# Where the last pass of a fused attention and mixture-of-experts kernel reads its eight tile numbers, transposes its first rows and signals the end of an expert

## The chip, the cores and the metric

The kernel runs on one core of a Trainium2 chip. The metric is the device time of one execution in microseconds, the median of several executions. One execution was also taken with the hardware profiler, and all rows below come from it.

A core has a matrix engine (PE; its weight loads are listed as PEld), a vector engine (DVE), a scalar engine (ACT), a general engine (POOL) and a queue engine (SP) that only starts transfers here. Each engine has a sequencer of its own, which reads its instructions in order; PEldq, DVEq, ACTq and SPq in a row stand for work of the sequencer alone: register arithmetic, branches, waits and loads of a number into a register.

## The reference

Three layers, in float32. N = 2304 tokens, width 512.

```python
scores = scale * np.matmul(q, k.transpose(0, 1, 3, 2))      # attention with a block mask
attn = np.exp(scores - max); attn = attn / (sum + 1e-9)
x = np.matmul(attn, v)                                      # to (2304, 512)
h = x @ w_in                                                # 512 -> 2048
x = np.maximum(0.01 * h, h) @ w_out                         # 2048 -> 512
do_compute = x @ w_skip > 0                                 # tokens that go to an expert
e_idx = np.argmax(x @ w_gate, axis=1)                       # one of 8 experts
h = np.maximum(xc[mask] @ w1[e], 0.0)                       # 512 -> 1024, expert e
y[mask] = gate_w[mask, None] * (h @ w2[e])                  # 1024 -> 512
out[do_compute] = xc + y                                    # the others keep x
```

## The kernel before, in words

Each engine has its own instruction list, and the lists meet only through semaphores: `wait_ge(s, n)` holds an engine until the counter `s` has reached `n`, and `then_inc` or `sem_inc` raises it. The order of the work is the order in which it is written.

Attention, the two projections and the gate take the first 640 us. After them the tokens of each expert lie in tiles of 128 rows. How many tiles an expert has is known only at run time. DVE therefore works out nine tile numbers (`base_i`, raised with `s_count`), and each engine reads all nine into registers: `tile_start(e, x)` is one such load, `tile_starts(e)` waits for `s_count` and does all nine. `starts[x]` to `starts[x + 1]` are then the bounds of a loop over the tiles of expert x, which each engine runs on its own. With this input the eight loops have 11 turns in all; the first expert has three, and one more tile, the early one, goes ahead of them.

- The **early tile** (`early_hidden`, `early_y`): PE multiplies its 128 tokens with both weights of expert 0. `early_y(f)`, f = 0 to 7, is one product of 512 columns, in `ps_y`; the last one raises `m_y` to 1.
- **A tile of the loops**, number g. POOL gathers its token rows from memory into `rows` (`m_gather`). PE transposes them (`transpose_rows(g)`, `m_rt`), DVE copies the transposed rows out of PSUM (`move_rows_t(g)`, L1286, `m_rows`), PE makes the hidden layer in two halves (L1612, `ps_hid`, `m_hid`), ACT rounds each half (`hid_hi`, `m_high`), DVE takes what rounding left (`hid_lo`, L1306, `m_low`), PE makes the second product out of hi and lo parts (L1623 to L1625, `ps_y`, `m_y`), DVE forms the result (`y_out`, `m_out`), POOL scatters it. The transposes of tile g + 1 stand between the two products of tile g.
- **Once for each expert** ACT rounds its second weight in four pieces (`high_w2`, L986), and DVE takes the rest in four pieces (`low_w2`, L1291). The rounded weight has one buffer for all experts, so ACT waits until the last product of the expert before is done, for which it reads `m_y`. At the same place it raises `s_expert`, on which SP waits before it loads the weights of expert x over those of x - 4. SP has two weight transfers under way at a time.

Of the kernel before, what the change touches and what calls it, by code (L numbers as in the profile page):

```python
# [15 lines left out]
P = 128  # L16
# [3 lines left out]
KC = DM // P  # L20
# [3 lines left out]
EC = F // P  # L24
# [121 lines left out]
def build(nc, q_t, k_t, v_r, w_in, w_out, w_gs, w1, w2, out):  # L146
    ctx = ExitStack()
    with ctx:
        def sb(name, shape, dt=F32, scope=ctx):
            return scope.enter_context(nc.sbuf_tensor(name, shape, dt))  # L150

        def ps(name, cols, scope=ctx):
            return scope.enter_context(nc.psum_tensor(name, [P, cols], F32))

        def sem(name):
            return ctx.enter_context(nc.semaphore(name))
# [6 lines left out]
        ident = sb("ident", [P, P])  # L163
# [104 lines left out]
        rows = sb("rows", [P, ROW_W])  # L268
# [30 lines left out]
        ps_rt = ps("ps_rt", BANK)  # L299
# [65 lines left out]
        s_ready = sem("s_ready")  # L365
        s_count = sem("s_count")
        s_order = sem("s_order")
        s_w = [[sem(f"s_w{i}{n}") for n in range(2)] for i in range(NW)]
        s_expert = sem("s_expert")
# [4 lines left out]
        m_gather = sem("m_gather")  # L374
        m_sidx = sem("m_sidx")
        m_scatter = sem("m_scatter")
        m_rt = sem("m_rt")
# [6 lines left out]
        m_y = sem("m_y")  # L384
# [85 lines left out]
        def loaded_to(e, x, n):  # L470

            for k, loaded in enumerate(s_w[x % NW]):
                e.wait_ge(loaded, 16 * (W_LOADS // 2 * (x // NW) + (n + 2 - k) // 2))
# [16 lines left out]
        def tile_start(e, x):  # L490
            return e.value_load(base_i[0:1, x:x + 1], min_val=0, max_val=MAX_TILES)

        def tile_starts(e):
            e.wait_ge(s_count, 1)
            return [tile_start(e, x) for x in range(E + 1)]
# [354 lines left out]
        def _(e):  # L850
# [77 lines left out]
            for s in range(STEPS):  # L928
# [14 lines left out]
                f, odd = divmod(s - 42, 2)  # L943
# [33 lines left out]
                e.copy(held[:, :], rows[:, :]).then_inc(m_held, 1)  # L977

            def high_w2(x, n):
                if n == 0 and x >= 1:  # L980

                    e.wait_ge(m_y, starts[x] + 1)
                    e.sem_inc(s_expert, 1)
                e.wait_ge(s_w2lo, W2_PIECES * x)
                loaded_to(e, x, KC + n)
                e.activation(w2_hi[:, 2 * n:2 * n + 2, :], w2_sb[x % NW][:, 2 * n:2 * n + 2, :], ACT.Copy).then_inc(s_w2hi, 1)  # L986
# [12 lines left out]
            starts = tile_starts(e)  # L999
# [17 lines left out]
        def _(e):  # L1017
# [266 lines left out]
            def move_rows_t(g):  # L1284
                e.wait_ge(m_rt, g + 1)
                e.tensor_copy(rows_t[:, :, :].rearrange("p k c -> p (k c)"), ps_rt[:, :]).then_inc(m_rows, 1)  # L1286

            def low_w2(x, n):
# [2 lines left out]
                e.tensor_tensor(w2_lo[x % NW][:, fs, :], w2_sb[x % NW][:, fs, :], w2_hi[:, fs, :].bitcast(F32),  # L1291
                                ALU.subtract).then_inc(s_w2lo, 1)

            starts = tile_starts(e)
            move_rows_t(0)
            e.wait_ge(m_y, 1)
            e.scalar_tensor_tensor(out=y_out[:, :], in0=ps_y[:, :], scalar=early[:, DM:DM + 1],
                                   in1=early[:, 0:DM], op0=ALU.mult, op1=ALU.add).then_inc(m_out, 1)
            for x in range(E):
                for n in range(W2_PIECES):  # L1300
                    low_w2(x, n)
                with e.Fori(starts[x], starts[x + 1]) as g:
                    for half in range(2):
                        fs = slice(EC // 2 * half, EC // 2 * (half + 1))
                        e.wait_ge(m_high, 2 * g + half + 2)
                        e.scalar_tensor_tensor(out=hid_lo[:, fs, :].rearrange("p f c -> p (f c)"), in0=ps_hid[half][:, :],  # L1306
                                               scalar=0.0, in1=hid_hi[:, fs, :].rearrange("p f c -> p (f c)").bitcast(F32),
                                               op0=ALU.max, op1=ALU.subtract).then_inc(m_low, 1)
                    move_rows_t(g + 1)
                    e.wait_ge(m_y, g + 2)  # L1310
                    e.wait_ge(m_kept, g + 2)
                    e.wait_ge(m_scatter, (g + 1) * 16)
                    e.scalar_tensor_tensor(out=y_out[:, :], in0=ps_y[:, :], scalar=kept[:, DM:DM + 1],
                                           in1=kept[:, 0:DM], op0=ALU.mult, op1=ALU.add).then_inc(m_out, 1)
# [3 lines left out]
        def _(e):  # L1318
# [221 lines left out]
                    if n % (EC // 2 * KC) == EC // 2 * KC - 1:  # L1540
                        last.then_inc(s_earlyhid, 1)

            def transpose_rows(g):
                e.wait_ge(m_gather, (g + 1) * 16)
                for c in range(KC):
                    last = e.transpose(ps_rt[:, P * c:P * c + P], rows[:, P * c:P * c + P], ident[:, :])
                last.then_inc(m_rt, 1)

            def early_y(f):

                if f == 0:
# [37 lines left out]
            tabulate(m)  # L1589
            early_hidden(27, EC * KC)  # L1590

            starts = []
            for f in range(EC):
                if f == EC - 1:
                    e.wait_ge(s_ready, 1)
                    transpose_rows(0)
                early_y(f)
                if f == 0:
                    e.wait_ge(s_count, 1)
                starts.append(tile_start(e, f))  # L1600
            starts.append(tile_start(e, E))

            for x in range(E):
                i = x % NW
                with e.Fori(starts[x], starts[x + 1]) as g:
                    e.wait_ge(m_rows, g + 1)
                    loaded_to(e, x, KC - 1)
                    e.wait_ge(m_low, 2 * g + 1)
                    for half in range(2):
                        for f in range(EC // 2 * half, EC // 2 * (half + 1)):  # L1610
                            for c in range(KC):
                                last = e.matmul(ps_hid[half][:, P * f - HALF * half:P * (f + 1) - HALF * half],  # L1612
                                                w1_sb[i][:, c, P * f:P * f + P], rows_t[:, c, :],
                                                start=c == 0, stop=c == KC - 1)
                        last.then_inc(m_hid, 1)
                    transpose_rows(g + 1)
                    e.wait_ge(m_out, g + 1)
                    for f in range(EC):
                        if f % 2 == 0:
                            e.wait_ge(s_w2lo, W2_PIECES * x + f // 2 + 1)  # L1620
                        if f % (EC // 2) == 0:
                            e.wait_ge(m_low, 2 * g + f // (EC // 2) + 2)
                        e.matmul(ps_y[:, :], hid_hi[:, f, :], w2_hi[:, f, :], start=f == 0, stop=False)  # L1623
                        e.matmul(ps_y[:, :], hid_hi[:, f, :], w2_lo[i][:, f, :], start=False, stop=False)  # L1624
                        last = e.matmul(ps_y[:, :], hid_lo[:, f, :], w2_hi[:, f, :], start=False, stop=f == EC - 1)  # L1625
                    last.then_inc(m_y, 1)


_NAMES = ("q_t", "k_t", "v_r", "w_in", "w_out", "w_gs", "w1", "w2")
# [24 lines left out]
```

## Time and profile before

| | |
|---|---|
| median of three executions | 800.74 us (799.68 to 808.11) |
| the profiled execution, its own time | 800.74 us |
| its span, first to last instruction | 798.5 us |
| PE busy | 762.1 us (95%) |
| DVE, ACT, POOL busy | 381.4, 308.4, 165.2 us |
| granted TensorE clock, mean | 0.997 of full speed |

The span is what the trace shows; the 2.2 us around it belong to the time as well. The profiled execution has the median's time. A busy share says only how much of the span an engine had work; what an edit is worth depends on which wait ends last at its place.

### The profile page before, as it was taken

To read this page: it belongs to the slowest core of one execution; us is meant where nothing else is said; L and a number is where in the kernel's file an instruction comes from. 1 tells how busy PE (TensorE), PEld (TensorE's weight loads), DVE (VectorE), ACT (ScalarE), POOL (GpSimd) and SP (SyncE) were. 2 spreads that over 40 slices of the span, in tenths; PEclk is the share of its full clock that TensorE was granted. 3 is DMA by queue.
4 is the path that set the end of the run, shared out by engine and by line. 5 is a ranking of instruction groups with operands and counts; after the bars stand their busy time and mean duration, and the time that the engine had idled before them with its cause. 6 is when DMAs were issued, how large, how long until landed. Compare 5 with 4: busy or idle time off the path is not lost.

```text
span 798.5 us, 13602 instructions
## 1 busy us (share of the span) xinstructions
PE 762.1 (95%) x4690; PEld 654.8 (82%) x4690; DVE 381.4 (48%) x790; ACT 308.4 (39%) x723; POOL 165.2 (21%) x201
## 2 busy tenths in 40 slices
PE   4887899999999999999999999999999999999997
PEld 3665688888988888899998778787787879999996
DVE  4878555543342464112344555655554341444554
ACT  3656656544443445334342222222321131333533
POOL 5344656321211223200020000000000032222222
PEclk9999999999999999999999999999999999999999
DMA  5646677754544443265766565565652137777750
GB/s 147 169 136 189 180 192 205 205 150 113 140 131 129 126 141 87 75 190 156 191 191 180 159 186 152 169 198 151 180 155 84 54 91 239 241 227 232 232 176 4
DMA packets 101623, 126.84 MB, mean 159 GB/s; under 512 B 15938, under 2 KB 62290, under 8 KB 101560
## 3 DMA queue, kind: packets, MB, share of 16 engines
q1 hardware_dynamic: 98392, 121.37, 52.3%
q0 software_dynamic: 2080, 3.77, 1.5%
q10 hardware_dynamic: 1088, 0.89, 0.5%
q8 instruction: 36, 0.59, 0.3%
q14 instruction: 27, 0.22, 0.1%
HBM read 92.89 MB, written 31.57 MB: 156 GB/s over the span
## 4 chain that ended last, share of the span: by engine, by line
PE 88%; DMA 4%; SPq 4%; issue 1%; ACT 1%; DVE 1%; POOL 0%; POOLq 0%; DVEq 0%; ACTq 0%
PE ps_hid L1612 10%; PE ps_h L1404 9%; PE ps_x L1454 9%; PE ps_x L1456 8%; PE ps_x L1455 8%; PE ps_h L1406 8%; PE ps_h L1405 8%; PE ps_o L1388 5%; PE ps_t L1362 3%; PE ps_y L1624 3%; PE ps_y L1625 3%; PE ps_y L1623 3%; PE ps_s L1347 2%; DMA k<-k_st 2%; PE ps_s L1348 2%
## 5 line engine op out<-in xcount | busy, mean ns | idle before, releaser
L1404 PE MATMUL ps_h<-xh,win_h 128*128 128x384 f32 x384 | 136.4, 355 | 3.0 <-ACT act L891 2.4
L1405 PE MATMUL ps_h<-xl,win_h 128*128 128x384 f32 x384 | 128.8, 336 | 0.0
L1406 PE MATMUL ps_h<-xh,win_l 128*128 128x384 f32 x384 | 128.8, 335 | 0.0
L1454 PE MATMUL ps_x<-wout_h,g_hi 128*128 128x512 f32 x288 | 117.0, 406 | 0.0
L1456 PE MATMUL ps_x<-wout_h,g_lo 128*128 128x512 f32 x288 | 112.5, 391 | 0.0
L1455 PE MATMUL ps_x<-wout_l,g_hi 128*128 128x512 f32 x288 | 112.2, 390 | 0.0
L891 ACT ACTIVATE act<-ps_h 128x384 f32<-128x384 f32 x96 | 47.1, 491 | 151.1 <-PE ps_h L1406 151.1
L1044 DVE COPY pt<-ps_t 128x256 f32<-128x256 f32 (+4 forms) x113 | 49.2, 443 | 107.0 <-PE ps_t L1362 106.8
L1078 DVE TENSOR_TENSOR g_lo<-g_raw,g_hi 128x512 fp32r<-128x512 f32 x72 | 49.6, 688 | 76.0 <-ACT g_hi L901 75.9
L879 ACT ACTIVATE prob<-ps_s,neg_max 128x128 f32<-128x128 f32 (+2 forms) x144 | 78.3, 547 | 9.3 <-DVE neg_max L1038 9.3
L1612 PEld LDWEIGHTS ps_hid<-rows_t,w_sb 128*128 128x128 f32 x704 | 80.2, 192 | 1.7 <-issue 0.8
L1404 PEld LDWEIGHTS ps_h<-xh,win_h 128*128 128x128 f32 x384 | 72.1, 188 | 10.8 <-issue 5.4
L1612 PE MATMUL ps_hid<-rows_t,w_sb 128*128 128x128 f32 x704 | 80.5, 275 | 0.0
L1038 DVE TENSOR_REDUCE neg_max<-ps_s 128x1 f32<-128x128 f32 (+2 forms) x144 | 71.7, 502 | 8.7 <-PE ps_s L1348 8.7
L705 POOL TENSOR_TENSOR k_st<-k_raw,k_st 64x576 fp32r<-64x576 f32 x32 | 45.6, 1426 | 142.6 <-DVE k_st L1024 142.3
L1405 PEld LDWEIGHTS ps_h<-xl,win_h 128*128 128x128 f32 x384 | 72.3, 188 | 0.0
L1406 PEld LDWEIGHTS ps_h<-xh,win_l 128*128 128x128 f32 x384 | 72.1, 188 | 0.0
L1456 PEld LDWEIGHTS ps_x<-wout_h,g_lo 128*128 128x128 f32 x288 | 54.1, 188 | 11.9
L1454 PEld LDWEIGHTS ps_x<-wout_h,g_hi 128*128 128x128 f32 x288 | 54.2, 188 | 11.7 <-issue 2.2
L1455 PEld LDWEIGHTS ps_x<-wout_l,g_hi 128*128 128x128 f32 x288 | 54.2, 188 | 9.5
L1347 PE MATMUL ps_s<-k_st,q_hi 128*128 128x128 f32 (+3 forms) x128 | 46.6, 364 | 15.5 <-POOL ident L733 10.8
L1362 PE MATMUL ps_t<-ident,prob 128*128 128x128 f32 x344 | 60.5, 279 | 0.7 <-ACT prob L879 0.7
(176 smaller groups left out, 1134.9 us busy)
## 6 DMA issues: line engine op xcount, KB each, us to landing
w_sb<-in_w SPq DMA_DIRECT2D x64, 512.0 KB, 5.4
hidden<-act SPq DMA_DIRECT2D x96, 192.0 KB, 2.5
g_raw<-hidden SPq DMA_DIRECT2D x72, 256.0 KB, 4.3
k_raw<-in_k_t SPq DMA_DIRECT2D x62, 144.0 KB, 3.0
q_raw<-in_q_t SPq DMA_DIRECT2D x32, 144.0 KB, 3.2
x2rows<-x SPq DMA_DIRECT2D x18, 256.0 KB, 2.5
out<-x SPq DMA_DIRECT2D x18, 256.0 KB, 2.7
k<-k_st SPq DMA_DIRECT2D x31, 144.0 KB, 2.8
```

The costliest lines, as they stand in the source:

```text
L879: e.activation(prob_of(u), score_out(u), ACT.Exp, bias=neg_max[:, u % 4:u % 4 + 1], scale=1.0, accum_out=row_sum[p % 2][:, i:i + 1]).then_ ...
L1038: e.tensor_reduce(out=neg_max[:, u % 4:u % 4 + 1], in_=src, axis=AX.XY if u % UNITS == TAIL else AX.X, op=ALU.max, negate=True).then_inc(s ...
L1078: e.tensor_tensor(g_lo[j % G_RING][:, :, :], g_raw[j % RAW_RING][:, :, :], g_hi[j % G_RING][:, :, :].bitcast(F32), ALU.subtract).then_inc( ...
L1347: e.matmul(dst, q_hi[h][:, P * qt:P * qt + P], k_st[h][:, 0:cols], start=True, stop=False)
L1362: last = e.transpose(t_bank(u, P, P * kt, P * kt + P), tile[:, P * kt:P * kt + P], ident[:, :])
L1404: e.matmul(dst, win_h[:, f, kc, :], xh[slot][:, kc, :], start=kc == 0, stop=False)
L1405: e.matmul(dst, win_h[:, f, kc, :], xl[slot][:, kc, :], start=False, stop=False)
L1406: last = e.matmul(dst, win_l[:, f, kc, :], xh[slot][:, kc, :], start=False, stop=kc == KC - 1)
L1454: e.matmul(dst, hi, wout_h[:, f, :], start=f == 0, stop=False)
L1455: e.matmul(dst, hi, wout_l[:, f, :], start=False, stop=False)
L1456: last = e.matmul(dst, lo, wout_h[:, f, :], start=False, stop=f == FC - 1)
L1612: last = e.matmul(ps_hid[half][:, P * f - HALF * half:P * (f + 1) - HALF * half], w1_sb[i][:, c, P * f:P * f + P], rows_t[:, c, :], start= ...
```

## The change

Three things.

1. PE now does the wait for `s_count` ahead of the first `early_y`, reads all its tile numbers behind the eight `early_y`, one behind each, and does the first `transpose_rows(0)` after all of these. Before, that transposition stood ahead of the last `early_y`.
2. DVE reads its nine tile numbers behind `move_rows_t(0)` and the first `y_out`. Before, it read them first of all.
3. The end of an expert is signalled by PE: behind the loop of each expert it waits until its own last product is done (`m_y`) and raises `s_expert`. ACT, which did both, now waits on `s_expert` ahead of each piece of `high_w2`.

```diff
@@ ACT
             def high_w2(x, n):
-                if n == 0 and x >= 1:
-                    e.wait_ge(m_y, starts[x] + 1)
-                    e.sem_inc(s_expert, 1)
+                e.wait_ge(s_expert, x)
                 e.wait_ge(s_w2lo, W2_PIECES * x)
@@ DVE
-            starts = tile_starts(e)
             move_rows_t(0)
             e.wait_ge(m_y, 1)
             e.scalar_tensor_tensor(out=y_out[:, :], in0=ps_y[:, :], scalar=early[:, DM:DM + 1],
                                    in1=early[:, 0:DM], op0=ALU.mult, op1=ALU.add).then_inc(m_out, 1)
+            starts = tile_starts(e)
             for x in range(E):
@@ PE
+            e.wait_ge(s_count, 1)
             starts = []
             for f in range(EC):
-                if f == EC - 1:
-                    e.wait_ge(s_ready, 1)
-                    transpose_rows(0)
                 early_y(f)
-                if f == 0:
-                    e.wait_ge(s_count, 1)
                 starts.append(tile_start(e, f))
             starts.append(tile_start(e, E))
+            e.wait_ge(s_ready, 1)
+            transpose_rows(0)
             for x in range(E):
...
                     last.then_inc(m_y, 1)
+                e.wait_ge(m_y, starts[x + 1] + 1)
+                e.sem_inc(s_expert, 1)
```

DVE's instructions from the last tile number worked out to the second weight of expert 0, before. TENSOR_LOAD with two ISA rows is one `tile_start`, and nine of them stand in a row.

```order
L1282 CAST base_i<-base_f 128x9 [waits s_t]
L491 TENSOR_LOAD base_i [waits s_count]
L491 ISA x2
...
L1286 COPY rows_t<-ps_rt 128x512 [waits m_rt]
L1297 SCALAR_TENSOR_TENSOR y_out<-ps_y,act 128x512 [waits m_y]
L1291 TENSOR_TENSOR w_lo<-w_sb,w_hi 128x1024 [waits s_w2hi] x4
```

The same place of the changed kernel:

```order
L1279 CAST base_i<-base_f 128x9 [waits s_t]
L1283 COPY rows_t<-ps_rt 128x512 [waits m_rt]
L1293 SCALAR_TENSOR_TENSOR y_out<-ps_y,act 128x512 [waits m_y]
L491 TENSOR_LOAD base_i [waits s_count]
L491 ISA x2
...
L1288 TENSOR_TENSOR w_lo<-w_sb,w_hi 128x1024 [waits s_w2hi] x4
```

The nine loads have moved from ahead of the copy and `y_out` to between `y_out` and the second weight's first piece.

PE's instructions from the last product of expert 0 to the first of expert 1, before. REGISTER_ALU and COMPARE_AND_BRANCH end the loop, the branch and the two ISA rows begin the next one.

```order
L1625 MATMUL ps_y<-w_hi,hid_lo 128x512
L1605 REGISTER_ALU
L1605 COMPARE_AND_BRANCH
L1605 UNCONDITIONAL_BRANCH
L1605 ISA
L1608 ISA [waits s_w11,s_w10,m_rows]
L1612 MATMUL ps_hid<-rows_t,w_sb 128x128 [waits m_low]
```

The same place of the changed kernel:

```order
L1620 MATMUL ps_y<-w_hi,hid_lo 128x512
L1600 REGISTER_ALU
L1600 COMPARE_AND_BRANCH
L1622 REGISTER_ALU
L1600 UNCONDITIONAL_BRANCH [waits m_y]
L1600 ISA
L1603 ISA [waits s_w11,s_w10,m_rows]
L1607 MATMUL ps_hid<-rows_t,w_sb 128x128 [waits m_low]
```

A wait on `m_y`, which the MATMUL four rows above it raises, now stands between the two products, at each of the eight ends of an expert.

## Rows read from the trace of the kernel before

**Rows 1.** The page, part 4: the chain that ended last, by engine.

```profile
PE 88%; DMA 4%; SPq 4%; issue 1%; ACT 1%; DVE 1%; POOL 0%; POOLq 0%; DVEq 0%; ACTq 0%
```

**Rows 2.** The view by stretches: from the second tile's first product to the last's.

```profile
core 0: us, PE busy (x) PEld busy (x) DVE busy (x) ACT busy (x) POOL busy (x), PEclk, DMA share, GB/s
661.78:780.04 118.26, 118.26 (x831) 108.83 (x830) 51.81 (x60) 43.08 (x60) 25.70 (x36) 1.00 0.70 224
```

**Rows 3.** The timeline from 640 to 656 us: start, length, engine, instruction.

```profile
640.30 0.60 ACT L990 ACTIVATE hid_early<-ps_hid 128x512 f32<-128x512 f32 x1 [3.51 <-PE ps_hid L1537]
...
647.55 0.69 DVE L1286 COPY rows_t<-ps_rt 128x512 f32<-128x512 f32 x1 [6.88 <-PE ps_rt L1546]
...
648.38 7.22 PEld L1612 LDWEIGHTS ps_hid<-rows_t,w_sb 128*128 128x128 f32 x64 [0.83 <-issue]
...
648.41 0.75 DVE L1297 SCALAR_TENSOR_TENSOR y_out<-ps_y,act 128x512 f32<-128x512 f32 x1 [0.17 <-PE ps_y L1556]
...
649.08 4.62 DVE L1291 TENSOR_TENSOR w_lo<-w_sb,w_hi 128x1024 fp32r<-128x1024 f32 x4
...
653.62 0.69 DVE L1306 SCALAR_TENSOR_TENSOR hid_lo<-ps_hid,hid_hi 128x512 fp32r<-128x512 f32 x1
...
655.96 0.19 PEld L1623 LDWEIGHTS ps_y<-w_hi,hid_hi 128*128 128x128 f32 x1
```

**Rows 4.** The chain from 640 us in order of time: start, length, what.

```profile
647.51 0.86 PE ps_y L1556 x2
648.38 7.41 PE ps_hid L1612 x64
...
780.04 7.14 PE ps_hid L1612 x64
```

**Rows 5.** Line L491, the register loads: ns min/median/max, first and last start us.

```profile
L491 ACTq TENSOR_LOAD <-base_i x9: 272/275/472, 640.7 to 645.2; - x9
...
L491 DVEq TENSOR_LOAD <-base_i x9: 297/304/547, 640.7 to 645.9; - x9
...
L491 DVEq SEQ_ASSERT  x9: 23/23/35, 641.5 to 646.5; - x9
```

**Rows 6.** The timeline of ACT and of DVE in the last tile.

```profile
780.24 3.90 ACT L986 ACTIVATE w_hi<-w_sb 128x1024 fp32r<-128x1024 f32 x4 [5.06 <-PE ps_y L1625]
...
783.61 2.35 DVE L1291 TENSOR_TENSOR w_lo<-w_sb,w_hi 128x1024 fp32r<-128x1024 f32 x2
...
787.85 0.69 DVE L1306 SCALAR_TENSOR_TENSOR hid_lo<-ps_hid,hid_hi 128x512 fp32r<-128x512 f32 x1 [1.29 <-ACT hid_hi L1010]
```

**Rows 7.** Sequencer work by line, columns as in Rows 5; x1: of a short stretch.

```profile
L1285 DVEq ALU_OP  x11: 40/40/40, 656.5 to 787.9; - x11
L1302 DVEq MOVE  x1: 36/36/36, 784.2 to 784.2; - x1
L983 ACTq EVENT_SEMAPHORE  x7: 17/17/17, 688.1 to 780.1; - x7
L1544 PEldq EVENT_SEMAPHORE  x1: 51/51/51, 645.7 to 645.7; - x1
L1605 PEldq MOVE  x8: 29/37/37, 647.2 to 776.0; - x8
L1608 PEldq FUSED_REGOPS  x11: 37/37/47, 648.3 to 776.3; - x11
```

**Rows 8.** The timeline of PE at 82 us, in the attention.

```profile
82.85 0.76 PE L1337 MATMUL ps_s<-k_st,q_hi 128*128 128x288 f32 x4 [3.73 <-DMA k<-k_st]
```

**Rows 9.** PE's waits over the whole span: total us, times, longest us.

```profile
PE ps_s L1337 <- DMA k<-k_st: 9.7, 4, 3.7
```

**Rows 10.** The view by stretches, the 4 us after that wait, columns as in Rows 2.

```profile
84.00:88.00 4.00, 4.00 (x19) 1.97 (x16) 1.85 (x5) 3.49 (x10) 3.14 (x3) 0.57 0.50 153
```

**Rows 11.** Line L592, all weight loads of the experts.

```profile
L592 SPq DMA_DIRECT2D w_sb<-in_w x64: 327/328/1269, 413.4 to 772.0; - x64
...
DMA to landing us min/median/max: 4.2/5.4/10.0
```

More of the change, by code:

```diff
@@ L1541, in early_hidden @@
                         last.then_inc(s_earlyhid, 1)
[L1543 to L1547, printed above, removed]
             def early_y(f):
@@ L1590, in _, with transpose_rows @@
             early_hidden(27, EC * KC)
+            e.wait_ge(s_count, 1)
             starts = []
             for f in range(EC):
-                if f == EC - 1:
-                    e.wait_ge(s_ready, 1)
-                    transpose_rows(0)
                 early_y(f)
-                if f == 0:
-                    e.wait_ge(s_count, 1)
                 starts.append(tile_start(e, f))
             starts.append(tile_start(e, E))
+            def transpose_rows(g):
+                e.wait_ge(m_gather, (g + 1) * 16)
+                for c in range(KC):
+                    last = e.transpose(ps_rt[:, P * c:P * c + P], rows[:, P * c:P * c + P], ident[:, :])
+                last.then_inc(m_rt, 1)
+            e.wait_ge(s_ready, 1)
+            transpose_rows(0)
             for x in range(E):
```

## The prediction, made before the changed kernel ran

> **What bounds the kernel now.** The chain that ended last is PE for 88% [rows 1], so I read next whether PE has any room where the change touches it. The view by stretches says no: from the second tile's first product to the last tile's PE is busy 118.26 us of 118.26 [rows 2], at the full clock. The reader is to see that here any time in which PE does nothing is added to the end, however short it is, unless a later wait would have eaten it. The expert pass has no such wait in PE's rows. Then I read the timeline around the first tile, for who releases whom [rows 3], the chain for what a product costs in the middle and after a pause [rows 4], and the sequencers' own rows, which busy time doesn't count [rows 5, 7], because two of the three edits move sequencer work and the third adds a sequencer wait.
>
> **1. PE's early tile.** Before, PE transposes the rows, then does the last `early_y`, and under that product (0.86 us in the chain, [rows 4]) DVE copies the rows out. The copy begins at 647.55 and takes 0.69; PE's first weight load of the hidden layer follows at 648.38, 0.83 behind the copy's start [rows 3]. That is nearly as long as the cover, so the copy costs little today. Afterwards all eight `early_y` come first, so the transposes end 0.86 later, and nothing stands on PE over the copy: its start moves to 647.55 + 0.86 = 648.41, PE's load to 648.41 + 0.83 = 649.24. The earlier wait on `s_count` adds a trifle. It is satisfied at about 640.7, when all sequencers begin to load [rows 5], and before it held the first register load, now the first `early_y` with that load right behind it; I put 0.05 us on it. The other loads run on PE's sequencer under the products, as they do now. Sum for this edit: 0.86 + 0.05 = **0.9 us**, all on the path.
>
> **2. DVE's nine loads.** They last from 640.7 to 646.5 [rows 5], 5.8 us. Before, they lie in DVE's wait of 6.88 us for the transposes [rows 3], so they cost nothing. What covers them is that wait, and the change takes them out of it. Behind them on DVE stand the four pieces of `w_lo` (649.08 to 653.62, where `hid_lo` follows at once) and then `hid_lo` of the first half, 0.69 us, for which PE's second product waits; PE came to it at 655.96 and did not have to wait [rows 3]: 655.96 - (653.62 + 0.69) = 1.65 us of room.
>
> When do the loads begin now? Two questions, two rows. Does DVE's sequencer pass an instruction whose wait isn't satisfied yet? The register step L1285 stands behind the second `hid_lo` of a tile, which waits for ACT; it ran at 787.9 in the last tile, where that `hid_lo` began at 787.85 after an idle 1.29 us [rows 6, 7]. It did not run during the idle time. So no: the loads can't begin before the copy is released. Does it run ahead of instructions that are released, but have not begun? The MOVE of L1302 behind the four pieces ran at 784.2 [rows 7], when ACT's fourth piece had just ended (780.24 + 3.90 = 784.14) and DVE was still in the third of its own (783.61 + 2.35 for two, [rows 6]). So yes. ACT's first load, too, ran at 640.7 while its activation of 640.30 to 640.90 was under way [rows 3, 5]. Hence the loads begin right behind the copy's release, at about 648.41 + 0.05 + 0.05 = 648.5, and end at 648.5 + 5.8 = 654.3. ACT's pieces are long done by then, so the four pieces take the same 653.62 - 649.08 = 4.54, `hid_lo` runs from 658.85 to 659.55, and PE starts its second product some 0.05 later, at 659.6, instead of 655.96. **The first tile ends 3.65 us later**; this holds the 0.9 us of the first edit, since PE would have been there at 655.96 + 0.9 = 656.9 and stands for 2.7 us. Bounds: if the loads had to wait until DVE has finished the copy and `y_out`, they begin 0.69 + 0.75 = 1.4 later, and the tile 5.1 us later. If they ran before the release they cost nothing, and only 0.9 is left. I take 3.65, which both rows speak for. What follows in the tile has room: the other half is due 12 products later.
>
> The Trainium skill speaks against this sum. Its page "Perfetto Trace Analysis", section "DVE / Act Engine Instruction (TENSOR_ADD, Activation, etc)", has the sequencer push an instruction into a wait queue and read on before its semaphores are satisfied. By that rule the loads would still run in DVE's long wait and the first tile would lose only the 0.9 us. The row on L1285 disagrees, and I go by the row.
>
> **3. The end of an expert.** Before, PE's sequencer is through the loop's end 4 us ahead of its array: the MOVE that opens the last loop ran at 776.0, the product behind it has its slot at 780.04 [rows 4, 7]. So all this branching is hidden under products. Now the sequencer has to stand until its own last product has reached PSUM. ACT saw the same event at 780.1 at the last such place, and the next product's slot began at 780.04 [rows 4, 7]. From there in order: PE's wait (51 ns each on this engine, with its spacing about 0.1), from MOVE to the last register step 776.3 - 776.0 = 0.3, from there to the weight load 648.38 - 648.3 = 0.1 [rows 3, 7]. Weight load at 780.6, 0.56 late. And the array starts empty, with a weight load that nothing covers: the first hidden layer, which came after such a pause, took 7.41 where a running one takes 7.14, 0.27 more [rows 4]. Together 0.83, of times given to a tenth, so I say **0.8 us**. ACT's semaphore row has seven such places in it [rows 7]; the eighth, behind the last expert, has no product behind it. 7 x 0.8 = **5.6 us**. Lower bound: PE loses at least the 0.27 and the 0.06 to the event and the 0.1 of its wait, 0.43 each, 3.0. Upper bound: reading new code behind the wait, which no row shows at this place; I allow the register part once more, 0.3 each, 7.7.
>
> Who else waits? ACT gets its signal about 0.1 us later than now, since PE passes it on, and its four extra waits lie under activations of one microsecond. DVE's chain has room: in the last tile the pieces end at 785.96 and `hid_lo` at some 786.6, while PE's hidden layer ends at 780.04 + 7.14 = 787.2, with transposes still to do [rows 4, 6], and PE comes later now. SP's weight loads wait on `s_expert` too. Even if the whole delay went into them, the last would land at 772.0 + 9.3 + 10.0 = 791.3 [rows 11]; its user is the fourth piece of ACT, at 780.24 + 3 x 0.95 + 9.3 = 792.4. So it costs nothing. Taking ACT's wait away gives nothing back, since ACT wasn't late.
>
> **Sum.** 3.65 + 5.6 = 9.25, say 9.3 us. The profiled execution took 800.74, which is also the median: 800.7 + 9.3 = **810.0 us**, span 807.8. About 1% is what a measurement of this kernel can tell from no change; its threshold is 808.7.
>
> **Rivals.**
> A. The sequencer passes unreleased waits, by whatever it does where no row looks: 0.9 + 5.6 = 6.5, 807.2. Against it L1285.
> B. The end of an expert is cheaper than I add up, at its lower bound: 3.65 + 3.0 = 6.7, 807.4. For it: a branch that overlaps the end of the product. Against it: the steps are in order on one sequencer.
> C. The stall of 2.7 us, or of 4.1 if the loads begin late, makes the TensorE clock drop. Once PE stood idle for 3.73 us, and in the 4 us from 84 on the granted clock was 0.57 in the mean, for most of them the lower of its levels, 1.2 instead of 2.4 GHz; that is 0.43 x 4 = 1.7 us of full clock. The three other waits of that kind were 6.0 us together [rows 8 to 10], and the mean clock of 0.997 over the span leaves no room for a drop behind each. So with the drop 810.0 + 1.7 = 811.7; with the late loads 811.7 + 1.4 = 813.1.
> D. Not slower: the stream of expert weights, not PE, sets the end of the pass, so that every pause of PE is paid back in a wait that gets shorter. It would give 800.7. It decides from the point where a weight lands later than PE needs it; the last was issued at 772.0 and lands in 10.0 at worst, before ACT's fourth piece at 783.1 [rows 6, 11], and PE has no idle time at all in [rows 2]. Nearly excluded.
>
> **Chances.** Forecast 0.62 (own range 808.3 to 811.3), A 0.10, B 0.08, C 0.17, D 0.03. The range reaches down to just under A and B and up over C with early loads: 806.6 to 812.4, leaving out D and the late end of C. Slower by over 1%: nearly all of the forecast and C, 0.76; within 1%: A, B, D and the low end of the forecast, 0.23; faster by over 1%: 0.01.
>
> **What would show it.** In the trace after: DVE's L491 loads from about 648.5 to 654.3, none before the copy; PE's L1607 load at 649.3 and L1618 load near 659.6, behind `hid_lo`; the tiles of one expert still 13.1 us apart, and 13.9 where an expert ends between them, seven times; ACT's and DVE's work unchanged in length. I am wrong if PE's second product of the first tile starts before 658, if the steps between experts are under 13.6 or over 14.2, or if a PE wait turns up on a weight load.

## The result and the profile after

| | before | after |
|---|---|---|
| median of 17 executions each | 804.37 us (799.68 to 810.79) | 815.15 us (808.83 to 820.58) |
| ratio after to before, 95% interval | | 1.0131 [1.0095, 1.0168] |
| the profiled execution, its own time | 800.74 us | 815.26 us |
| its span | 798.5 us | 813.0 us |
| PE busy | 762.1 us | 769.2 us |
| granted TensorE clock over the span, mean | 0.997 | 0.988 |

The change makes the kernel slower by 1.3%. The forecast was +9.3 us, a ratio of 1.012. The ratio of 1.0131 on the median of 804.37 is +10.5 us, and the two medians lie 10.8 apart. The absolute forecast of 810.0 us and its range up to 812.4 were missed, because they stood on 800.7 for the kernel before, and its median over 17 executions is 804.4.

The profile of the changed kernel. The page, busy time and chain by engine, to be read beside [rows 1]:

```profile
PE 769.2 (95%) x4690; PEld 657.4 (81%) x4690; DVE 380.3 (47%) x790; ACT 309.1 (38%) x723; POOL 165.3 (20%) x201
...
PE 85%; SPq 4%; DMA 4%; issue 2%; DVE 2%; ACT 1%; POOL 1%; DVEq 1%; POOLq 0%; ACTq 0%
```

PE's share of the chain fell from 88% to 85%, and DVE, its sequencer and "issue" have a percent more each: the path to the end now leaves PE in places where it did not before.

The timeline around the first tile, to be read beside [rows 3]. Everything here starts some 5 us later than in the profile before; that arises ahead of everything that the change touches (below), so I read distances from the first row, in which DVE writes the tile numbers.

```profile
645.16 0.17 DVE L1279 CAST base_i<-base_f 128x9 int32<-128x9 f32 x1
...
653.09 0.69 DVE L1283 COPY rows_t<-ps_rt 128x512 f32<-128x512 f32 x1 [7.75 <-PE ps_rt L1593]
653.70 0.74 DVE L1293 SCALAR_TENSOR_TENSOR y_out<-ps_y,act 128x512 f32<-128x512 f32 x1
653.92 7.22 PEld L1607 LDWEIGHTS ps_hid<-rows_t,w_sb 128*128 128x128 f32 x64 [1.10 <-issue]
...
659.22 4.63 DVE L1288 TENSOR_TENSOR w_lo<-w_sb,w_hi 128x1024 fp32r<-128x1024 f32 x4 [4.78 <-issue]
663.77 1.28 DVE L1303 SCALAR_TENSOR_TENSOR hid_lo<-ps_hid,hid_hi 128x512 fp32r<-128x512 f32 x2
...
664.51 0.19 PEld L1618 LDWEIGHTS ps_y<-w_hi,hid_hi 128*128 128x128 f32 x1 [2.98 <-DVE hid_lo L1303]
664.51 0.50 PE L1618 MATMUL ps_y<-w_hi,hid_hi 128*128 128x512 f32 x1 [2.74 <-DVE hid_lo L1303]
```

Line L491, DVE's register loads, to be read beside [rows 5]:

```profile
L491 DVEq TENSOR_LOAD <-base_i x9: 298/311/555, 653.1 to 658.6; - x9
...
L491 DVEq SEQ_ASSERT  x9: 23/23/35, 653.9 to 659.1; - x9
```

The reader is to see the "4.78 <-issue" on `w_lo`: DVE's array stands still, waits for nothing that another engine owes it, and all the while its own sequencer loads numbers (653.1 to 659.1). Then `hid_lo` comes late and PE stands 2.74 us for it.

The chain at the ends of experts, start, length and what, to be read beside [rows 4], and PE's row for the new wait:

```profile
670.34 7.14 PE ps_hid L1607 x64
...
683.47 7.14 PE ps_hid L1607 x64
...
696.62 0.57 issue
697.19 7.41 PE ps_hid L1607 x64
...
710.59 0.57 issue
711.16 7.41 PE ps_hid L1607 x64
```

```profile
L1623 PEldq EVENT_SEMAPHORE  x8: 51/51/51, 696.6 to 807.8; - x8
```

The tiles of the first expert follow each other at once (670.34, 683.47: 13.13 apart, hidden layer 7.14). At an end of an expert stand 0.57 of "issue" and a hidden layer of 7.41. The view of waits for the same stretch sums it up (us in total, times, longest):

```profile
PE ps_hid L1607 <- PE ps_y L1620: 4.1, 7, 0.6
...
PE ps_y L1618 <- DVE hid_lo L1303: 2.7, 1, 2.7
```

**Where the time went.** To compare kernels whose expert pass begins at different times, I take one distance in every trace: from the start of `base_i` to the start of the last `y_out`. I call it the pass. Before it was 793.34 - 640.50 = 152.84 us:

```profile
640.50 0.17 DVE L1282 CAST base_i<-base_f 128x9 int32<-128x9 f32 x1
...
793.34 0.75 DVE L1313 SCALAR_TENSOR_TENSOR y_out<-ps_y,kept 128x512 f32<-128x512 f32 x1 [4.20 <-PE ps_y L1625]
```

After it is 807.85 - 645.16 = 162.69. The change therefore costs **9.85 us** in the rows, and the spans differ by 14.5 only because the profiled execution after reached `base_i` 4.66 later, in work that the change does not touch.

### The profile page after: what moved, and what is told of

Read it like the earlier page. It is cut to its first block, busy times and chain, and to the rows that moved or that the text cites. A ratio compares the mean times of both kernels' runs of the same rounds, so it can differ in the third digit from the quotient of the medians.

```text
span 813.0 us, 13636 instructions
## 1 busy us (share of the span) xinstructions
PE 769.2 (95%) x4690; PEld 657.4 (81%) x4690; DVE 380.3 (47%) x790; ACT 309.1 (38%) x723; POOL 165.3 (20%) x201
## 4 chain that ended last, share of the span: by engine, by line
PE 85%; SPq 4%; DMA 4%; issue 2%; DVE 2%; ACT 1%; POOL 1%; DVEq 1%; POOLq 0%; ACTq 0%
PE ps_hid L1607 9%; PE ps_x L1451 9%; PE ps_h L1401 9%; PE ps_x L1453 8%; PE ps_x L1452 8%; PE ps_h L1402 8%; PE ps_h L1403 8%; PE ps_o L1385 6%; PE ps_t L1359 3%; PE ps_y L1618 3%; PE ps_y L1620 3%; PE ps_y L1619 3%; PE ps_s L1344 2%; DMA k<-k_st 2%; PE ps_s L1345 2%
## 5 line engine op out<-in xcount | busy, mean ns | idle before, releaser
L1401 PEld LDWEIGHTS ps_h<-xh,win_h 128*128 128x128 f32 x384 | 72.1, 188 | 10.5 <-issue 4.7
```

The costliest lines, as they stand in the source:

```text
L1401: e.matmul(dst, win_h[:, f, kc, :], xh[slot][:, kc, :], start=kc == 0, stop=False)
```

## The experiments

All kernels start from the kernel before unless another is named. "Hidden" and "second" are PE's first hidden-layer load and its first second-product load of tile 0, counted from the start of `base_i`; "pass" is the distance above; "clock 0:100" is the granted clock in the first 100 us of the span.

| kernel | `base_i` | clock 0:100 | hidden | second | pass | over before | ratio of times [95%] |
|---|---|---|---|---|---|---|---|
| before | 640.50 | 0.98 | 7.88 | 15.46 | 152.84 | | |
| before_again | 644.49 | 0.91 | 7.79 | 15.37 | 152.76 | -0.08 | 0.9982 [0.9947, 1.0017] |
| after | 645.16 | 0.91 | 8.76 | 19.35 | 162.69 | 9.85 | 1.0131 [1.0095, 1.0168] |
| after_again | 646.48 | 0.90 | 8.67 | 19.26 | 162.63 | 9.79 | 1.0110 [1.0068, 1.0152] |
| pe_order | 650.22 | 0.86 | 8.66 | 16.24 | 153.63 | 0.79 | 1.0016 [0.9980, 1.0051] |
| dve_loads | 644.15 | 0.93 | 7.79 | 19.25 | 158.00 | 5.16 | 1.0084 [1.0046, 1.0122] |
| expert_end | 649.42 | 0.86 | 7.79 | 15.37 | 158.79 | 5.95 | 1.0081 [1.0050, 1.0112] |
| pe_dve | 640.27 | 0.98 | 8.66 | 19.26 | 158.24 | 5.40 | 1.0077 [1.0040, 1.0114] |
| pe_dve_again | 643.57 | 0.93 | 8.66 | 19.25 | 156.68 | 3.84 | one execution |
| met_wait | 646.01 | 0.91 | 7.79 | 15.37 | 152.80 | -0.04 | 1.0011 [0.9974, 1.0048] |
| every_tile | 640.32 | 0.97 | 7.79 | 15.36 | 164.11 | 11.27 | 1.0160 [1.0095, 1.0224] |
| fill_pauses | 648.64 | 0.95 | 7.78 | 15.36 | 152.80 | -0.04 | 1.0055 [1.0022, 1.0088] |
| early_cover | 643.94 | 0.95 | 6.94 | 15.09 | 152.47 | -0.37 | 0.9994 [0.9964, 1.0023] |

In the first profile of the kernel before, "hidden" is 7.88; in the six others that leave PE's early tile as it was it is 7.78 or 7.79. So a difference from that first profile is good to 0.1 us.

### pe_order: the first edit alone

```diff
+            e.wait_ge(s_count, 1)
             for f in range(EC):
-                if f == EC - 1:
-                    e.wait_ge(s_ready, 1)
-                    transpose_rows(0)
                 early_y(f)
-                if f == 0:
-                    e.wait_ge(s_count, 1)
                 starts.append(tile_start(e, f))
             starts.append(tile_start(e, E))
+            e.wait_ge(s_ready, 1)
+            transpose_rows(0)
```

> The kernel before with edit 1 alone: PE waits for s_count first, does all eight early_y and then the first transposes; DVE and the expert ends as before. I measure the expert stretch, from the start of DVE's last tile-number step (CAST base_i) to the start of the last y_out; it was 152.84 us before (640.50 to 793.34) and is 162.69 after the change (645.16 to 807.85). My theory (three local causes that add up): the stretch grows by 0.9 us, all of it ahead of the first hidden-layer product, so 153.7. Rival (the excess over the forecast comes from the code being laid out differently, anywhere): the stretch stays within 0.1 of a kernel without the edit and the time ahead of it moves. The whole time: within 1% of before.

Measured: the hidden layer begins 0.78 later from `base_i` (8.66 for 7.88), and the pass is 0.79 longer; 153.7 was expected, 153.63 measured. The timeline of this kernel:

```profile
658.06 0.69 DVE L1286 COPY rows_t<-ps_rt 128x512 f32<-128x512 f32 x1 [7.66 <-PE ps_rt L1546]
...
658.88 7.22 PEld L1610 LDWEIGHTS ps_hid<-rows_t,w_sb 128*128 128x128 f32 x64 [1.10 <-issue]
```

The load starts 0.82 behind the copy's start, nearly as before (0.83), but the product that used to run over the copy now lies ahead of it. By time alone the edit can't be told from nothing (1.0016).

### dve_loads: the second edit alone

```diff
-            starts = tile_starts(e)
             move_rows_t(0)
             e.wait_ge(m_y, 1)
             e.scalar_tensor_tensor(out=y_out[:, :], in0=ps_y[:, :], ...).then_inc(m_out, 1)
+            starts = tile_starts(e)
```

> The kernel before with edit 2 alone: DVE reads its nine tile numbers behind the first y_out. The transposes are released at 647.55 as before, so the loads run for 6.0 us (653.1 to 659.1 in the changed kernel) from there, w_lo starts at 653.6 instead of 649.08, the first hid_lo ends near 658.8 and PE, which came at 655.96, stands for 2.9 us. My theory: the stretch is 152.84 + 2.9 = 155.7. Rival (a sequencer reads past a wait that isn't met): loads while DVE waits, stretch 152.84. Second rival (the stall makes the TensorE clock drop): a lower granted clock in the 10 us behind the stall and a stretch of about 157.4.

Timeline and line L491 of this kernel:

```profile
644.15 0.17 DVE L1282 CAST base_i<-base_f 128x9 int32<-128x9 f32 x1
...
651.11 0.69 DVE L1286 COPY rows_t<-ps_rt 128x512 f32<-128x512 f32 x1 [6.78 <-PE ps_rt L1546]
...
651.97 0.75 DVE L1296 SCALAR_TENSOR_TENSOR y_out<-ps_y,act 128x512 f32<-128x512 f32 x1 [0.17 <-PE ps_y L1556]
...
658.11 4.63 DVE L1291 TENSOR_TENSOR w_lo<-w_sb,w_hi 128x1024 fp32r<-128x1024 f32 x4 [5.39 <-issue]
...
663.40 0.80 PE L1623 MATMUL ps_y<-w_hi,hid_hi 128*128 128x512 f32 x1 [3.61 <-DVE hid_lo L1306]
```

```profile
L491 DVEq TENSOR_LOAD <-base_i x9: 296/310/576, 652.0 to 657.5; - x9
```

The pass of 158.00 missed the expected 155.7 by 2.3 us. The second product comes 3.79 late, a microsecond more than this edit's share of the forecast, which is 3.65 less the 0.9 of the first edit; the other 1.37 is a drop of the clock (below, at pe_dve). The loads did not begin behind the copy (651.11) but at 652.0, when `y_out` was released. In PE's old order the last `early_y`, for which `y_out` waits, ends 0.86 behind the copy's release; in the new order it ends ahead of it. So the loads begin 7.9 us behind `base_i` with or without the first edit, and the second product comes 19.25 or 19.26 behind it. **The two edits do not add**: 0.78 and 3.79 alone, 3.80 together.

These rows also decide whether the sequencer passes an instruction whose wait is unmet. DVE waited 6.78 us for the transposes with the loads third in its list, the tile numbers were ready (PE's own loads of them began at 644.4), and not one load ran until both waits ahead were satisfied; then the first of them began, under the execution of `y_out`.

### expert_end: the third edit alone

```diff
@@ ACT
-                if n == 0 and x >= 1:
-                    e.wait_ge(m_y, starts[x] + 1)
-                    e.sem_inc(s_expert, 1)
+                e.wait_ge(s_expert, x)
@@ PE
                     last.then_inc(m_y, 1)
+                e.wait_ge(m_y, starts[x + 1] + 1)
+                e.sem_inc(s_expert, 1)
```

> The kernel before with edit 3 alone: PE waits for its own last product at the end of each expert and raises s_expert; ACT waits on s_expert. My theory: each of seven ends costs 0.84 us (0.57 of pause and 0.27 of a product that starts from an empty array, as in the changed kernel), stretch 152.84 + 5.9 = 158.7. Rival (in the changed kernel part of the cost came from ACT or DVE being late after the first tile's stall): under 0.6 each, stretch below 157. If edits 1 and 2 give 0.9 and 2.9, then the three sum to 9.7 against 9.85 measured.

The chain of this kernel, at the last of seven such ends ("issue" is 0.56 to 0.60 at all seven):

```profile
794.06 0.59 issue
794.65 7.41 PE ps_hid L1609 x64
```

The pass is 5.95 longer and the first tile unchanged; 5.95 / 7 = 0.85 for each end. Sum of the parts: 3.80 + 5.95 = 9.75, and the whole change measured 9.85 and 9.79. No part of the change gives anything back.

### before_again: the same kernel once more

> The kernel before, unchanged, timed and profiled once more. In the changed kernel's profile the stretch accounts for 9.85 us of the 14.5 us between the spans; the other 4.66 lie ahead of it, in code that the change doesn't touch, with 17 us at half clock in the first 100 us where the profile of before has 3.4. My theory (that part is chance, from run to run): the unchanged kernel shows it too: its stretch is 152.8 again, while its start of the stretch differs from 640.5 by some microseconds and follows the granted clock of the first 100 us. Rival (the change caused it): the stretch starts at 640.5 within 0.5 again.

The view by stretches, 0 to 100 us, of the kernel before and of this run (columns as in [rows 2]), and the timeline's row of `base_i` in this run:

```profile
0.00:100.00 100.00, 74.49 (x479) 57.18 (x481) 67.12 (x155) 57.46 (x162) 47.65 (x58) 0.98 0.59 164
```

```profile
0.00:100.00 100.00, 76.08 (x448) 57.14 (x449) 64.74 (x149) 53.45 (x151) 44.95 (x55) 0.91 0.55 152
```

```profile
644.49 0.17 DVE L1282 CAST base_i<-base_f 128x9 int32<-128x9 f32 x1
```

The program is the same; one execution got through 479 matmuls in the first 100 us at a clock of 0.98, the other through 448 at 0.91, and reached `base_i` 3.99 later. The pass itself is the same to 0.08. So two profiled executions of one kernel differ by 4 us ahead of the change's place, and the profile on which I forecast was the earlier of the two.

The traces also show where the difference arises. In none of the thirteen profiles is the clock under 1.00 between 100 us and `base_i`, and in the first 100 us it is so only in stretches that begin within 2 us of the end of one of the four pauses that PE makes between 38 and 92 us, waits for `k` as in [rows 8] (three of the four in fill_pauses have another cause). In the first profile of the kernel before, the pauses of 2.16, 1.98 and 1.83 us had no such stretch behind them and the one of 3.73 us had [rows 10]. In pe_order, whose program is the same up to there, the pauses were 2.11, 2.44, 2.27 and 2.90 us, and the view by stretches behind the four is:

```profile
40.40:44.40 4.00, 4.00 (x17) 3.35 (x19) 1.49 (x4) 2.10 (x6) 1.18 (x2) 0.50 0.31 97
57.40:61.40 4.00, 4.00 (x17) 3.33 (x19) 1.51 (x4) 2.17 (x7) 1.25 (x2) 0.50 0.30 87
74.20:78.20 4.00, 3.97 (x17) 3.36 (x19) 1.46 (x4) 2.16 (x7) 0.87 (x3) 0.50 0.51 146
92.00:96.00 4.00, 4.00 (x17) 3.30 (x19) 1.54 (x4) 3.25 (x9) 2.83 (x4) 0.50 0.39 108
```

All four run at the lower level, 1.2 GHz, and that execution reached `base_i` 9.72 us later than the first.

### pe_dve and pe_dve_again: the first two edits together, twice

> The kernel before with edits 1 and 2 together, expert ends as before. Alone, edit 1 made the stretch 153.62 (0.8 more) and edit 2 made it 158.00 (5.2 more, of which PE's second product starts 3.8 later, and the rest is a half-clock interval behind a pause of 3.6 us). My theory now: edit 2 alone has its loads held not by the copy but by y_out, whose release is the last early_y, 0.86 after the transposes; edit 1 puts y_out's release ahead of the copy's, so that the two together cost less than edit 2 alone: PE's second product 19.3 us after CAST base_i, a pause of 2.7 us, stretch 152.84 + 3.9 = 156.8, no half clock behind it. Rival (the costs add up): 0.8 + 3.8 = 4.6, stretch 157.4 or more, pause 3.6.

> The kernel with edits 1 and 2, one more profile. By the theory that the pause of 2.7 us drops the clock only in some executions: stretch 158.2 with a half-clock interval in the expert pass, or 156.8 (steps of y_out 17.0 instead of 18.4 at the first tile) without one. Either way PE's second product 19.26 us after CAST base_i.

Both have the second product at 19.25 or 19.26, as expected, and PE's pause of 2.75 and 2.74. But the pass was 5.40 longer in one (158.24 for the expected 156.8) and 3.84 in the other. The view by stretches behind the pause, first of pe_dve, then of pe_dve_again:

```profile
661.00:665.00 4.00, 4.00 (x12) 3.12 (x11) 0.00 (x0) 0.00 (x0) 0.06 (x1) 0.57 0.85 261
```

```profile
664.00:668.00 4.00, 4.00 (x19) 3.23 (x18) 0.00 (x0) 0.00 (x0) 0.35 (x2) 1.00 0.79 254
```

In the first the clock was 0.57 in the mean, 1.2 GHz for most of those 4 us (12 matmuls for 19); in the second it stayed at 1.00. That is 5.40 - 3.84 = 1.56 us. In dve_loads, where PE stood 3.61, it fell too (0.58 in the mean from 663.4 to 667.0): 5.16 - 3.79 = 1.37 of that kernel's pass. In the two profiles of the whole change it stayed at 1.00. A drop behind the pause of 2.7 us was seen in one of four profiles.

### met_wait and every_tile: what the end of an expert costs by itself

Both add to the kernel before a wait and a signal that nobody needs, the first of an event that is long past, the second behind every tile of its own last product.

```diff
@@ PE, met_wait: behind the loop of each expert
+                e.wait_ge(m_y, starts[x + 1])
+                e.sem_inc(s_idle, 1)
@@ PE, every_tile: last in the body of the loop
                     last.then_inc(m_y, 1)
+                    e.wait_ge(m_y, g + 2)
+                    e.sem_inc(s_idle, 1)
```

> The kernel before, to which PE does at each expert's end the same steps as in edit 3, a register step, a wait on m_y and a sem_inc (on a semaphore that nobody reads), but waits for one tile less, starts[x + 1] instead of starts[x + 1] + 1, which has been done for 13 us. ACT signals s_expert as before. It tells the drain from the steps. My theory (PE has to stand until its own last product has come out, and the loop's steps then stand bare): nothing, steps of 13.14 between all tiles, stretch 152.8. Rival (the added instructions, or code fetched anew, cost on their own): 0.2 to 0.84 at each of seven ends, stretch 154 to 158.7.

> The kernel before, to which PE waits for its own last product at the end of every tile instead of every expert (m_y at g + 2, then a sem_inc nobody reads). ACT signals s_expert as before, so that ACT isn't in the relay. Ten ends have a product behind them instead of seven. My theory: 0.84 us each, 8.4 in all, stretch 161.2, also in the first expert, whose three tiles are 13.13 apart today and then 13.97. Rival (it is the start of a new loop, not the drain, that costs): nothing at the turns inside a loop; ends of experts 0.84, stretch 158.7. Since the turn of a loop has fewer steps than the start of one, a turn may be up to 0.2 cheaper.

The chain of met_wait, whose third row is the first tile behind the end of an expert, then of every_tile:

```profile
667.25 7.14 PE ps_hid L1613 x64
...
680.39 7.14 PE ps_hid L1613 x64
...
693.52 7.14 PE ps_hid L1613 x64
```

```profile
648.11 7.41 PE ps_hid L1613 x64
...
661.52 0.98 issue
662.50 7.41 PE ps_hid L1613 x64
...
675.91 0.85 issue
676.76 7.41 PE ps_hid L1613 x64
```

With a wait that is already met the tiles stay 13.13 apart and the pass is unchanged, though there are as many added instructions as in expert_end. With the wait on its own product inside the loop, ten places cost 11.27, 1.13 each, for the expected 0.84. So what costs is the standstill: PE's array runs empty, and the wait, the registers and the branch come one after the other behind the last product. All ten places are dearer than the 0.56 to 0.60 of "issue" in expert_end: 0.98, 0.85 and 0.86 at the three turns inside a loop, 0.79 to 0.96 at the seven ends of experts. Here the loop's own counting and branching stand behind the wait (661.7 and 661.9 in PE's sequencer, the wait at 661.5), while in expert_end they stand ahead of it. That this order makes the difference is read from the rows; no kernel changed it alone.

### fill_pauses: something for PE to do in the attention's pauses

```diff
@@ PE, scores(u): ahead of the waits for the next head's k
+                if i == TAIL and 1 <= p <= 4:
+                    e.wait_ge(s_exp, s_freed(u))
+                    c = BANK * (s_slot(u) % S_RING)
+                    for _ in range(8):
+                        e.matmul(ps_s[:, c:c + P], ident[:, :], ident[:, :], start=True, stop=True)
```

The added products compute nothing that is used.

> The kernel before, with eight unneeded 128-column products of ident on PE ahead of the wait for k in four places of the attention (pairs 1 to 4, first step of the fifth unit), into a score bank that is free and overwritten next. In all profiles so far these are the four places where PE pauses for 1.8 to 3.7 us, and the half-clock intervals of the first 100 us (3.4 to 27 us in sum) begin behind them. My theory (these pauses, and where the clock's own time grid lies against them, make the start of the expert stretch vary from 640.5 to 650.2): shorter pauses of at most 1 us, no half clock in the first 100 us, CAST base_i at 640 or a little earlier, and a median some 4 us under before. Rival (the intervals come from the thin load there, not from the pauses): half clock as before, CAST base_i at 644 to 652, the products cost up to 1.8 x 4 = 7 us more.

PE's waits in the first 150 us (L1325 is the added line):

```profile
PE ps_s L1325 <- ACT prob L879: 5.8, 3, 2.5
...
PE ps_s L1342 <- DMA k<-k_st: 2.8, 1, 2.8
```

It failed to fill the pauses. The added products stand at 27.1, 42.2, 58.8 and 74.7 us. At the first of these PE had no pause before, at the other three they wait for ACT (1.81, 1.53 and 2.50 us) as the old ones waited for the transfer, and the last old pause was not touched (2.82 us for `k`). The lower clock stood behind the 1.81 and the 2.82. The kernel got slower (1.0055) where it was to gain 4 us; the added products took 9.7 us of PE's rows. One thing did change: its twelve executions had mean clocks of 0.990 to 0.995, while 13 of the 29 of the kernel before in the same job lay below 0.990, down to 0.981. That fits the pauses as the place where the clock falls, but which pause lowers it in which execution is not settled.

### after_again: the changed kernel once more

> The changed kernel, unchanged, timed and profiled once more. In its first profile the pause of 2.74 us in the first tile had no half clock behind it and the stretch was 162.69; edits 1 and 2 alone, with the same pause (2.75 us), had a half-clock interval of 3.4 us behind it and 1.5 us more stretch than the 156.8 I expected. My theory: the pause can drop the clock or not, from run to run, so this profile shows either 162.7 or some 164.2, nothing between; steps of 13.97 to 14.02 at seven ends and 13.13 to 13.15 elsewhere in both cases. The whole time: 9.8 to 11.3 us over before, ratio 1.012 to 1.014. Rival (edit 3 keeps the clock up somehow, or edits 1 and 2 without it differ): never a drop, 162.7 again; one more profile without a drop wouldn't settle it.

Pass 162.63 for 162.69, hidden, second and pause equal to 0.1, no drop of the clock behind the pause, ratio 1.0110 [1.0068, 1.0152]. The intervals of both timings hold 1.0122, which is 9.85 us on a median of 804 to 807.

### early_cover: the first edit in the other direction

The transposes go one product earlier, ahead of `early_y(6)`, so that two products run over the copy.

```diff
-                if f == EC - 1:
+                if f == EC - 2:
                     e.wait_ge(s_ready, 1)
                     transpose_rows(0)
                 early_y(f)
-                if f == 0:
+                if f == 1:
                     e.wait_ge(s_count, 1)
-                starts.append(tile_start(e, f))
+                if f >= 1:
+                    starts.append(tile_start(e, f - 1))
+            starts.append(tile_start(e, E - 1))
```

> The kernel before with the opposite of edit 1: transpose_rows(0) one early_y earlier (ahead of f = 6 instead of f = 7), and the register loads one early_y later, so that the second early_y doesn't wait for the first load. Two small pauses of PE in before: 0.55 us ahead of the second early_y and 0.27 at the first hidden layer. My theory: both go, the first hidden-layer load comes 7.05 us after CAST base_i instead of 7.88, stretch 152.0, the whole time 0.8 us less, 0.1%, which the timing can't tell from nothing but the stretch can. Rival (the loads then end after PE's early products and hold the first hidden layer; or the gathered rows are not there yet): stretch 152.8 or more.

The hidden layer began 0.85 to 0.94 earlier (6.94), but the pass is only 0.37 shorter. PE's timeline shows who took the rest:

```profile
658.64 0.66 PE L1546 MATMUL ps_rt<-ident,rows 128*128 128x128 f32 x4 [0.35 <-DMA rows<-x2rows,gather_at]
```

PE, earlier now, had to wait 0.35 for the gathered rows of the second tile, and the transposes behind that wait took 0.66, where the chain gives them 0.44 in the kernel before: 0.57 of the gain is gone. The expected 152.0 was missed, for the reason that the rival had named. The ratio of 0.9994 [0.9964, 1.0023] is no measurable gain.

## Why the prediction was right and wrong

**The step that failed is the base**, the first term of the sum, which was put at 800.7 and given no spread. "The profiled execution took 800.74, which is also the median: 800.7 + 9.3". The median was one of three executions that lay 8.4 us apart (799.68 to 808.11), nearly the size of the forecast difference. Over 17 executions it is 804.37, and it was 802.60, 805.08 and 807.15 in the three jobs of the experiments. The profile said which kind of execution it was: its mean clock of 0.997. For rival C the prediction had read that the clock fell behind one of PE's four waits for `k`, and that 0.997 leaves no room for more; it did not ask for another execution, and in pe_order it fell behind all four, with 9.72 us until `base_i`. Executions are listed with that clock, and their times fall in step with it:

| mean granted clock | before, median us (count) | after, median us (count) | difference |
|---|---|---|---|
| 0.995 and more | 799.36 (21) | 809.35 (3) | 10.0 |
| 0.990 to 0.994 | 802.58 (18) | 813.59 (7) | 11.0 |
| 0.987 to 0.989 | 805.07 (22) | 815.56 (5) | 10.5 |
| 0.983 to 0.986 | 807.90 (26) | 817.11 (4) | 9.2 |
| 0.980 to 0.982 | 809.85 (4) | 820.21 (5) | 10.4 |

(All executions of the two kernels whose clock is on record, 91 and 24; one of 1772.87 us of the kernel before is left out.) A straight line through each kernel's points, with one slope for both, puts the changed kernel 10.0 us above the other at equal clock, with a standard error of 0.24.

A forecast of 804.4 + 9.3 = 813.7 would have been 1.5 us low. The range had no term for the base at all. Those three executions alone spread 7.4 us upward from the value taken; with that added the range would have held the time. The mechanism came out as forecast: steps of 13.97 to 14.02 us at the seven ends, the second product behind `hid_lo`, no wait of PE on a weight.

**1. PE's early tile.** Forecast 0.9, measured 0.78 against the first profile of the kernel before and 0.87 against the usual 7.79. Right, for the stated reason: the product that covered the copy is gone.

**2. DVE's nine loads.** Their start was forecast at 648.5, 8.0 behind `base_i`; they began 7.9 behind it. Their length was 6.0 for 5.8 (653.1 to 659.1). The four pieces and `hid_lo` behind them took as long as forecast, and the second product came 19.35 - 15.46 = 3.89 late for 3.65; the pause of PE was 2.74 for 2.7. Right, and 0.2 short, nearly all of it the loads' length. What the forecast did not see is that this number holds without the first edit too. It read the edits as 0.9 and a rest, and the second edit alone costs 3.79.

Rival A is out: no load ran in 7.75 us of waiting, and the first began when the copy did (653.1, 653.09). The Trainium skill, page "Perfetto Trace Analysis", section "DVE / Act Engine Instruction (TENSOR_ADD, Activation, etc)", has the sequencer decode the next instruction while the one before sits in a wait queue with its semaphores unmet. By that rule the loads would have cost nothing here. The measurement decides against it for these instructions. Running ahead of instructions that are released but not finished was seen as forecast: the first loads went under the copy and `y_out`.

**3. The end of an expert.** Forecast 7 x 0.8 = 5.6, measured 7 x 0.85 = 5.95: "issue" 0.57 for 0.56, and the empty array's 0.27, as read from [rows 4]. The rounding down from 0.83 to 0.8 made most of the 0.35. Rival B (0.43 each) is out, met_wait shows that the added instructions by themselves cost nothing, and every_tile that the standstill does. Nobody else was late: there is no wait of PE on a weight transfer between 640 and 812 us.

**Rival C** was right for some executions. One profile in four showed the drop behind the pause, at 1.56 us for the forecast 1.7. Rows give 9.85 for a pass without a drop, and times at equal clock 10.0. The recorded ratio gives 10.5. A drop in some of the executions lowers their mean clock too and would fill part of that 0.65; so would chance in the medians. Which executions had one can't be read from their times, so this share is argued, not shown.

**Rival D** is out: no pause was paid back.

**What stays open** is why the clock falls behind a pause in one execution and not in another. That is what moves `base_i` by up to 10 us (640.3 to 650.2) in kernels that are the same up to there: it goes with the granted clock of the first 100 us, 0.98 to 0.86 (fill_pauses apart), all of whose low stretches stand at PE's four pauses, and the unchanged kernel alone shows 4 us of it.

## What to carry to other kernels

Work of an engine's sequencer (register loads, here nine in 6.0 us) is free while the engine has released work to run, as PE's loads under the `early_y`, or while it waits for someone else, if it stands ahead of that wait in its list. Behind the wait, on an engine with little left to run, it is a stall, and everything queued behind it is late. An engine that always has work should not wait for its own last result: let the one who needs the event wait for it. And before a difference of 1% is forecast as an absolute time, look at the clock at which the profiled execution ran, and give the base a term of its own in the range.

## What the runs showed of the hardware

- A wait on a semaphore that is already met costs PE nothing, even between two tiles (met_wait, -0.04 us for seven of them in the pass). A wait on its own product cost 0.85 us (expert_end), and 1.13 in every_tile, where the loop's branch stands behind it.
- The TensorE clock behind equal pauses of PE (2.74 and 2.75 us, same program) fell in one execution and stayed in another (pe_dve, pe_dve_again). Behind PE's pauses for `k` it fell after 2.11 us in pe_order and not after 2.16 us in the kernel before.
- Executions of the unchanged kernel lie up to 13 us apart (797.88 to 810.72 where the clock is on record), in step with the clock they were granted: from the group at 0.995 and more to that at 0.980 to 0.982 it is 10.5 us.
- DVE's sequencer did no register load in 7.75 us of an unmet wait ahead of it, and began the first of nine (653.1) when the copy ahead of it began (653.09).
